# Expert tiles of a fused attention, routed-expert and gated-layer kernel: the turns of the inner rows are placed among the products

## The chip, the cores and the metric

The kernel runs on one core of one Trainium2 chip. The metric is the device time of one execution in microseconds (us); lower is better. Before the change it is 1116.9 us, the median of three runs. A time of another kernel is compared with runs of this one on the same chip.

## The reference

Three stages follow one another. Only the second is touched.

```python
state = gamma[None, :, None, None] * state + np.einsum('bhd,bhe->bhde', k[:, :, t], v[:, :, t])
y[:, :, t] = scale * np.einsum('bhd,bhde->bhe', q[:, :, t], state)
...
logits = x @ w_gate                      # x: 3072 x 512, 8 experts
e_idx = np.argmax(logits, axis=1)
for e in range(E):
    mask = e_idx == e
    h = np.maximum(x[mask] @ w1[e], 0.0) # w1[e]: 512 x 1024
    ye = h @ w2[e]                       # w2[e]: 1024 x 512
    out[mask] = gate_w[mask, None] * eom[mask, e, None] * ye
...
xn = x / rms * rms_g
g = xn @ w_gate
return (silu(g) * (xn @ w_val) @ w_out)  # inner width 1536
```

The second stage sends each of the 3072 rows through the one expert that it scores highest.

## The kernel before

Every float32 product is made of three matmuls: each operand is split into a high part in a shorter format and the low remainder, and high x high, high x low and low x high are summed in one PSUM bank. ScalarE copies out the high part (a cast), VectorE subtracts it for the low part.

The rows are sorted by expert into tiles of 128 rows. Here there are 29 real tiles, numbered 0 to 28. Tiles 0 and 1 (LEAD) are written out, since the table that steers the others is not known yet: VectorE makes it in a long chain of small operations (lines 1188 to 1291) while those two tiles run. Tiles 2 to 21 run in a hardware loop (line 695), 22 and 23 are written out, and 24 to 28 run in loops in which each pass asks whether the tile is real (lines 707 to 713). The loop on each engine has its own control instructions, and the engines meet through semaphores.

On TensorE a tile a is: `up` (line 617), 12 matmuls for inner columns 0 to 511 (g = 0) and 12 for 512 to 1023 (g = 1); `turn_hidden`, which turns the inner rows `hid` by identity matmuls, 4 for g = 0, then `turn_rows(a + 1)` (line 608), which turns the 4 blocks of the next tile's gathered rows `xg`, then 4 for g = 1 (line 632); `down_tile` (line 644), 24 matmuls, 12 for each g in the order w2h x hidh, w2l x hidh, w2h x hidl. So a tile has 48 products of 512 columns and 12 turns of 128 columns.

Around that, ScalarE makes `hid` from each half of `up` (`relu`, line 852), then `hidh` for g = 0 (line 869), `xgh` of the next tile's rows (`rows_hi`, line 859) and `hidh` for g = 1. VectorE makes `hidl` for g = 0 (line 1163), `xgl` (`rows_lo`, line 1158), `hidl` for g = 1. GpSimd gathers the rows two tiles ahead once `tile_turned` says that `xg` is free.

The weights of the next expert are split while the present one's tiles run. In the first tile of an expert ("go") ScalarE splits three pieces (line 821) between `tile_result` of the tile before and `relu(a, 0)`, and one piece at the tile's end; in the second tile ("held") the same with the four pieces of w2. VectorE makes their low parts (line 1128).

Waits of TensorE that bear on the change: `relu_done` before each `turn_hidden` half, `hTh` (hidh is there) and `hTl` (hidl is there) in `down_tile`, `rows_in` before `turn_rows`, `tileT_lo` (xgl is there) at the next tile's head.

Of the kernel before, what the change touches and what calls it, by code (L numbers as in the profile page):

```python
# [16 lines left out]
P = 128  # L17
# [14 lines left out]
SURE = TOKENS // P  # L32
# [68 lines left out]
def build(nc, q, k, v, w_gate, w_og, w1, w2, f_gate, f_val, f_out, rms_g, out):  # L101
    with ExitStack() as ctx:
# [16 lines left out]
        s = {n: ctx.enter_context(nc.semaphore(n)) for n in sem_names}  # L119
# [156 lines left out]
        def quad(b):  # L276
            return bank[b][:, :].rearrange("p (a b) -> p a b", b=P)
# [200 lines left out]
        def _(pe):  # L478
# [123 lines left out]
            def turn_rows(a):  # L602

                pe.wait_ge(s["rows_in"], 16 * (a + 1))
                if not (isinstance(a, int) and a < 1):
                    pe.wait_ge(s["tileT_lo"], a)
                for i in range(KD):
                    mm = pe.transpose(quad(XG_T)[:, i, :], xg[:, i * P:(i + 1) * P], ident)  # L608
                mm.then_inc(s["tile_turned"], 1)

            def up(a, at, g):

                if not (isinstance(a, int) and a == 0):
                    pe.wait_ge(s["relu_done"], 2 * a - 1 + g)
                terms = [(x, wt, i) for x, wt in ((xgh, w1h), (xgh, w1l), (xgl, w1h)) for i in range(KD)]
                for n, (x, wt, i) in enumerate(terms):
                    mm = pe.matmul(bank[(UP0, UP1)[g]][:, :], x[:, i, :], wt[:, ds(at + (i * FE + g * 512), 512)],  # L617
                                   start=(n == 0), stop=(n == len(terms) - 1))
                mm.then_inc(s["up_done"], 1)

            def turn_hidden(a):

                first = isinstance(a, int) and a == 0
                for g in range(2):
                    if g:
                        turn_rows(a + 1)
                    pe.wait_ge(s["relu_done"], 2 * a + g + 1)
                    if not first:
                        pe.wait_ge(s["hTl"], 2 * a - 1 + g)
                    for i in range(4):  # L630
                        f = 4 * g + i
                        mm = pe.transpose(quad((HT0, HT1)[g])[:, i, :], hid[:, f * P:(f + 1) * P], ident)  # L632
                    mm.then_inc(s["h_turned"], 1)

            def down_tile(a, at):

                if not (isinstance(a, int) and a == 0):
                    pe.wait_ge(s["tile_out"], a)
                for g in range(2):
                    for x, wt in ((hidh, w2h), (hidh, w2l), (hidl, w2h)):  # L640
                        if wt is w2h:
                            pe.wait_ge(s["hTh" if x is hidh else "hTl"], 2 * a + g + 1)
                        for f in range(4 * g, 4 * g + 4):
                            mm = pe.matmul(bank[DOWN][:, :], x[:, f, :], wt[:, ds(at + f * D, D)],  # L644
                                           start=(f == 0 and x is hidh and wt is w2h),
                                           stop=(f == KE - 1 and x is hidl))
                mm.then_inc(s["tiles_done"], 1)

            def expert_tile(a):
                at = pe.value_load(run_at[0:1, ds(a, 1)], min_val=0, max_val=HALF)  # L650
                run = pe.value_load(run_of[0:1, ds(a, 1)], min_val=0, max_val=EXPERTS - 1)
                pe.wait_ge(s["tileT_lo"], a + 1)
                pe.wait_ge(s["lo_done"], RUN * run + PER)
                for g in range(2):
                    up(a, at, g)
                turn_hidden(a)
                pe.wait_ge(s["lo_done"], RUN * run + RUN)
                down_tile(a, at)

# [8 lines left out]
            gate_logits(last)  # L668
            pe.wait_ge(s["x_out"], last)
            turn_x(last)  # L670
            up(0, 0, 1)
            ranks(last)
            turn_hidden(0)
            pe.wait_ge(s["xT_out"], UNITS)
            down_tile(0, 0)
            for a in range(1, LEAD):
                pe.wait_ge(s["tileT_lo"], a + 1)
                for g in range(2):
                    up(a, 0, g)
                turn_hidden(a)  # L680
                down_tile(a, 0)
            def turn_xn(n, halves):

# [40 lines left out]
            def weights_ready(n, m, f):  # L724

                if isinstance(n, int) and n == 0:
                    if needs_piece(m, f):
                        pe.wait_ge(s["lo_done"], RUN * runs + needs_piece(m, f))
                    else:
                        pe.wait_ge(s["early_done"], 2)  # L730

            def gate_value(n, f):
                g = NF * n + f
                if f >= 2 or not (isinstance(n, int) and n == 0):
                    pe.wait_ge(s["prod_done"], g - 1)
                for m in range(2):
                    weights_ready(n, m, f)
                    for i in range(KD):
                        if f == 0 and m == 0:
                            pe.wait_ge(s["xl_ready"], KD * n + i + 1)  # L740
                        mm = three(bank[GV[f % 2][m]][:, :], gate_parts(m, f, i),
                                   (xh[:, i, :], xl[:, i, :]), i == 0, i == KD - 1)
                mm.then_inc(s["gv_done"], 1)
# [37 lines left out]
        def _(act):  # L781
# [66 lines left out]
            def relu(a, g):  # L848
                act.wait_ge(s["up_done"], 2 * a + g + 1)
                if g == 0 and not (isinstance(a, int) and a < 1):  # L850
                    act.wait_ge(s["h_turned"], 2 * a)
                nc.scalar.activation(hid[:, g * 512:(g + 1) * 512], bank[(UP0, UP1)[g]][:, :], ACT.Relu)\  # L852
                  .then_inc(s["relu_done"], 1)

            def rows_hi(a):
                act.wait_ge(s["tile_turned"], a + 1)
                if not (isinstance(a, int) and a < 1):
                    act.wait_ge(s["up_done"], 2 * a)
                nc.scalar.activation(xgh[:], quad(XG_T), ACT.Copy).then_inc(s["tileT_hi"], 1)

            def turned_hi_parts(a):

                for g in range(2):
                    if g:
                        rows_hi(a + 1)
                    act.wait_ge(s["h_turned"], 2 * a + g + 1)
                    if g == 0 and not (isinstance(a, int) and a < 1):
                        act.wait_ge(s["tiles_done"], a + 1)
                    nc.scalar.activation(hidh[:, 4 * g:4 * g + 4, :], quad((HT0, HT1)[g]), ACT.Copy).then_inc(s["hTh"], 1)  # L869

            def tile_result(a):
                act.wait_ge(s["tiles_done"], a + 2)
# [23 lines left out]
            def expert_tile(a, numbers=None):  # L896
                is_go, is_held, turn, to = numbers or tile_numbers(a)
                tile_result(a - 1)

                with act.If(is_go):  # L900
                    split_run_hi(turn, to, range(EARLY))
                with act.If(is_held):
                    split_run_hi(turn, to, range(PER, HELD_EARLY))
                relu(a, 0)
                store_tile(a - 1)
                relu(a, 1)
                turned_hi_parts(a)
                with act.If(is_go):
                    split_run_hi(turn, to, range(EARLY, PER))
                    with act.If(act.value_load(whole[0:1, ds(a, 1)], min_val=0, max_val=1)):  # L910
                        split_run_hi(turn, to, range(PER, RUN))
                with act.If(is_held):
                    split_run_hi(turn, to, range(HELD_EARLY, RUN))
# [2 lines left out]
            evacuate_yT(UNITS - 1)  # L916
            relu(0, 0)
            evacuate_x(UNITS - 1)
            relu(0, 1)
            turned_hi_parts(0)  # L920
            for a in range(1, LEAD):
                tile_result(a - 1)
                relu(a, 0)
                relu(a, 1)
                turned_hi_parts(a)
                put_tile(a - 1, (a - 1) * P)
            exps()
# [120 lines left out]
        def _(dve):  # L1048
# [107 lines left out]
            def rows_lo(a):  # L1156
                dve.wait_ge(s["tileT_hi"], a + 1)
                v3.tensor_tensor(xgl[:], quad(XG_T), xgh[:].bitcast(F32), ALU.subtract).then_inc(s["tileT_lo"], 1)
# [5 lines left out]
                  .then_inc(s["hTl"], 1)  # L1164

            def turned_lo_parts(a):
                for g in range(2):
                    if g:
                        rows_lo(a + 1)
                    hidden_lo_part(a, g)  # L1170

            choose(UNITS - 2)
            rows_lo(0)
# [141 lines left out]
                    split_run_lo(RUN * (run + 1), to, range(HELD_EARLY, RUN))  # L1315

            for a in range(1, LEAD):
                rows_lo(a + 1)
                hidden_lo_part(a, 1)
            gates_of_rows()  # L1320
            for i in range(PRE_A, PRE):
                split_pre_lo(i)
# [312 lines left out]
```

## Time and profile before

| | |
|---|---|
| median of 3 runs | 1116.9 us (1116.73 to 1118.97) |
| time of the profiled execution | 1117.19 us |
| its span | 1115.4 us |
| TensorE busy | 1093.2 us, 98% of the span |
| VectorE, ScalarE, GpSimd busy | 441.2, 377.8, 176.9 us |
| chain that ended last | TensorE 92%, VectorE 3%, DMA 2%, issue 2% |

The profiled execution is 0.3 us above the median of the runs. Stages on the span: attention and routing to about 145 us, the expert tiles to about 514.5 us, the gated layer after that. TensorE is busy nearly throughout, so a change can give back only the short times in which it waits between its matmuls, and can lose by making it wait anew.

### The profile page before, as it was taken

The page shows a single profiled execution, that of the slowest core. Times are in us where ns is not written, and L with a number is a line of the kernel's source. Part 1 is how long each engine was busy: PE and PEld are TensorE (multiplying, and loading weights), DVE is VectorE, ACT ScalarE, POOL GpSimd, SP SyncE. Part 2 cuts the span into 40 slices and gives each one's busy share as a digit, 9 for nine tenths or more (in the row PEclk, how much of TensorE's full clock was granted, in tenths as well). Part 3 has the DMA queues.
Part 4 walks back from the last instruction along what each step waited for, and adds up shares of the span by engine and source line. Part 5 has one row for each costly group of instructions (what it writes and reads, how often), then busy time and mean ns, then how long its engine had stood idle before and what let it go on. Part 6 is the DMA issues. An engine that isn't in the chain of part 4 may idle for free.

```text
span 1115.4 us, 20314 instructions
## 1 busy us (share of the span) xinstructions
PE 1093.2 (98%) x6307; PEld 908.0 (81%) x6308; DVE 441.2 (40%) x868; ACT 377.8 (34%) x613; POOL 176.9 (16%) x245
## 2 busy tenths in 40 slices
PE   7999999999999999999999999999999999999998
PEld 6888888888888888787888888788878878887886
DVE  4777767332414425432433333423333242333222
ACT  3545435343525446432224231231133122212112
POOL 2444423322221201000000300200030011001000
PEclk9999999999999999999999999999999999999999
DMA  9999816434445533422201210111021001101001
GB/s 216 243 252 240 245 61 211 148 113 122 113 122 168 172 122 133 153 76 97 63 6 34 76 35 4 47 28 38 0 75 26 12 38 38 38 0 38 1 1 38
DMA packets 114068, 101.52 MB, mean 91 GB/s; under 512 B 81856, under 2 KB 87392, under 8 KB 114016
## 3 DMA queue, kind: packets, MB, share of 16 engines
q1 hardware_dynamic: 98752, 66.07, 22.2%
q0 software_dynamic: 8832, 26.81, 7.7%
q10 hardware_dynamic: 6432, 7.96, 2.0%
q8 instruction: 31, 0.51, 0.2%
q14 instruction: 21, 0.17, 0.1%
HBM read 76.41 MB, written 20.22 MB: 87 GB/s over the span
## 4 chain that ended last, share of the span: by engine, by line
PE 92%; DVE 3%; DMA 2%; issue 2%; ACT 1%; POOL 0%; SPq 0%; POOLq 0%; ACTq 0%; DVEq 0%
PE bank L720 14%; PE bank L722 14%; PE bank L721 14%; PE banks L644 14%; PE bank L617 14%; PE banks L720 3%; PE banks L722 3%; PE banks L721 3%; PE bank L528 2%; PE banks L514 2%; PE bank L558 1%; DMA x_rows<-x_out,slot_idx 1%; PE banks L632 1%; PE bank L608 1%; PE bank L632 1%
## 5 line engine op out<-in xcount | busy, mean ns | idle before, releaser
L1397 DVE TENSOR_TENSOR gated<-bank,sig 128x512 f32<-128x512 f32 x72 | 49.8, 692 | 344.1 <-ACT sig L1011 344.1
L1011 ACT ACTIVATE sig<-bank 128x512 f32<-128x512 f32 x72 | 43.1, 598 | 328.9 <-PE bank L722 328.9
L720 PE MATMUL bank<-xh,w1h 128*128 128x512 f32 x384 | 149.4, 389 | 0.0
L721 PE MATMUL bank<-xl,w1h 128*128 128x512 f32 x384 | 149.4, 389 | 0.0
L722 PE MATMUL bank<-xh,w1l 128*128 128x512 f32 x384 | 149.4, 389 | 0.0
L721 PEld LDWEIGHTS bank<-xl,w1h 128*128 128x128 f32 x384 | 72.1, 188 | 15.0
L722 PEld LDWEIGHTS bank<-xh,w1l 128*128 128x128 f32 x384 | 72.1, 188 | 15.0
L720 PEld LDWEIGHTS bank<-xh,w1h 128*128 128x128 f32 x384 | 72.1, 188 | 14.9
L1018 ACT ACTIVATE hh<-prod 128x512 fp32r<-128x512 f32 x72 | 45.5, 632 | 110.7 <-DVE prod L1401 110.7
L1163 DVE TENSOR_TENSOR hidl<-bank,hidh 128x512 fp32r<-128x512 f32 x29 | 20.0, 691 | 131.8 <-ACT hidh L869 131.8
L1406 DVE TENSOR_TENSOR hl<-prod,hh 128x512 fp32r<-128x512 f32 x72 | 49.9, 692 | 54.2 <-ACT hh L1018 54.2
L1598 POOL DMA_INDIRECT out_rows<-x_out,cur_idx x10 | 10.1, 1007 | 380.4 <-ACT x_out L1025 290.0
L644 PE MATMUL banks<-w2h,hidh 128*128 (+1 forms) x232 | 64.8, 401 | 0.4
L617 PE MATMUL bank<-w1h,xgh 128*128 (+1 forms) x232 | 62.7, 392 | 1.3 <-issue 1.3
L1128 DVE TENSOR_TENSOR w1l<-stage,w1h 128x1024 f32 (+1 forms) x40 | 48.1, 1232 | 39.7 <-ACT w1h L821 39.7
L644 PE MATMUL banks<-w2h,hidl 128*128 (+1 forms) x232 | 62.2, 390 | 0.0
L644 PE MATMUL banks<-w2l,hidh 128*128 (+1 forms) x232 | 62.2, 390 | 0.0
L617 PE MATMUL bank<-w1h,xgl 128*128 (+1 forms) x232 | 62.2, 390 | 0.0
L617 PE MATMUL bank<-w1l,xgh 128*128 (+1 forms) x232 | 62.0, 389 | 0.0
L852 ACT ACTIVATE hid<-bank 128x512 f32<-128x512 f32 x58 | 34.4, 594 | 79.9 <-PE bank L617 79.9
L1503 POOL DMA_INDIRECT xg<-x_rows,cur_idx x28 | 28.6, 1022 | 206.4 <-PE bank L608 204.7
L720 PE MATMUL banks<-w2h,hh 128*128 128x512 f32 x144 | 56.8, 394 | 4.4 <-DVE hl L1406 4.4
(243 smaller groups left out, 2130.6 us busy)
## 6 DMA issues: line engine op xcount, KB each, us to landing
stage<-in_moe_w SPq DMA_DIRECT2D x64, 512.0 KB, 5.6
expert_rows<-tile_o ACTq DMA_DIRECT2D x29, 256.0 KB
q_raw<-in_q SPq DMA_DIRECT2D x24, 256.0 KB, 6.0
k_raw<-in_k SPq DMA_DIRECT2D x24, 256.0 KB, 6.5
v_raw<-in_v SPq DMA_DIRECT2D x24, 256.0 KB, 4.6
stage<-stage SPq DMA_DIRECT2D x64, 64.0 KB, 2.0
stage<-in_moe_w_out SPq DMA_DIRECT2D x6, 512.0 KB, 4.1
stage<-in_moe_w_gate SPq DMA_DIRECT2D x5, 512.0 KB, 5.4
```

The source lines that it names most:

```text
L617: mm = pe.matmul(bank[(UP0, UP1)[g]][:, :], x[:, i, :], wt[:, ds(at + (i * FE + g * 512), 512)], start=(n == 0), stop=(n == len(terms) - 1))
L644: mm = pe.matmul(bank[DOWN][:, :], x[:, f, :], wt[:, ds(at + f * D, D)], start=(f == 0 and x is hidh and wt is w2h), stop=(f == KE - 1 and ...
L720: pe.matmul(out_ap, lh, rh, start=first, stop=False)
L721: pe.matmul(out_ap, lh, rl, start=False, stop=False)
L722: return pe.matmul(out_ap, ll, rh, start=False, stop=last)
L852: nc.scalar.activation(hid[:, g * 512:(g + 1) * 512], bank[(UP0, UP1)[g]][:, :], ACT.Relu)\
L1011: nc.scalar.activation(sig[:], bank[GV[f % 2][0]][:, :], ACT.Sigmoid).then_inc(s["sig_done"], 1)
L1018: nc.scalar.activation(hh[:, f % 2, :], prod[:], ACT.Copy).then_inc(s["hid_hi"], 1)
L1128: nc.vector.tensor_tensor(into[:, ds(at, PIECE)], stage[:, i % STAGE, :], hi[:, ds(at, PIECE)].bitcast(F32), ALU.subtract).then_inc(s["lo_ ...
L1397: v3.tensor_tensor(gated[:], bank[GV[f % 2][0]][:, :], sig[:], ALU.mult).then_inc(s["gated_done"], 1)
L1406: v3.tensor_tensor(hl[:, f % 2, :], prod[:], hh[:, f % 2, :].bitcast(F32), ALU.subtract)\
L1503: nc.gpsimd.indirect_dma_start(xg[:].bitcast(U32), None, x_dram, bass.IndirectOffsetOnAxis(cur_idx[:, 0:1], 0))\
```

## The change

On TensorE the 4 turns of g = 0 move from behind the `up` products into the middle of those of g = 1; the 4 turns of g = 1 move behind the first four `down` products; the turns of the next tile's rows move between the two halves of `down`. ScalarE makes `relu(a, 1)` after `hidh` of g = 0, and `rows_hi(a + 1)` last. VectorE makes `rows_lo(a + 1)` last. The bank of the turned rows is used again by the gated layer, so that layer's first use of it gets a wait. The numbers of operations are the same.

```diff
-            def up(a, at, g):
+            def up(a, at, g, between=None):
...
                 for n, (x, wt, i) in enumerate(terms):
+                    if between and n == len(terms) // 2:
+                        between()
...
             def down_tile(a, at):
 
                 if not (isinstance(a, int) and a == 0):
                     pe.wait_ge(s["tile_out"], a)
                 for g in range(2):
                     if g:
                         turn_rows(a + 1)
...
                     for x, wt in ((hidh, w2h), (hidh, w2l), (hidl, w2h)):
+                        if not g and x is hidh and wt is w2l:
+                            turn_hidden(a, 1)
...
-                for g in range(2):
-                    up(a, at, g)
-                turn_hidden(a)
+                up(a, at, 0)
+                up(a, at, 1, lambda: turn_hidden(a, 0))
                 pe.wait_ge(s["lo_done"], RUN * run + RUN)
                 down_tile(a, at)
...
+                    if isinstance(n, int) and n == 0 and GV[f % 2][m] == XG_T and f < 2:
+                        pe.wait_ge(s["tileT_lo"], extra + SURE + 1)
+                        pe.sem_inc(s["stood"], 1)
...
                 for g in range(2):
                     if g:
-                        rows_hi(a + 1)
+                        relu(a, 1)
                     act.wait_ge(s["h_turned"], 2 * a + g + 1)
...
+                rows_hi(a + 1)
...
             def turned_lo_parts(a):
-                for g in range(2):
-                    if g:
-                        rows_lo(a + 1)
-                    hidden_lo_part(a, g)
+                hidden_lo_part(a, 0)
+                hidden_lo_part(a, 1)
+                rows_lo(a + 1)
...
             for a in range(1, LEAD):
+                hidden_lo_part(a, 1)
                 rows_lo(a + 1)
-                hidden_lo_part(a, 1)
```

TensorE, tile 1, from the `up` products of g = 1 (`w1h,xgh` and so on are the three terms; `con,hid` is a turn of inner rows, `con,xg` of the next rows), before:

```order
L617 MATMUL bank<-w1h,xgh 128x512 [waits relu_done]
L617 MATMUL bank<-w1h,xgh 128x512 x3
L617 MATMUL bank<-w1l,xgh 128x512 x4
L617 MATMUL bank<-w1h,xgl 128x512 x4
L632 MATMUL bank<-con,hid 128x128 [waits hTl,relu_done]
L632 MATMUL bank<-con,hid 128x128 x3
L608 MATMUL bank<-con,xg 128x128 [waits tileT_lo,rows_in]
L608 MATMUL bank<-con,xg 128x128 x3
L632 MATMUL banks<-con,hid 128x128 [waits hTl,relu_done]
L632 MATMUL banks<-con,hid 128x128 x3
L644 MATMUL banks<-w2h,hidh 128x512 [waits hTh,tile_out]
L644 MATMUL banks<-w2h,hidh 128x512 x3
```

The same place in the changed kernel, from the fifth of those twelve products on:

```order
L619 MATMUL bank<-w1l,xgh 128x512 x2
L630 MATMUL bank<-con,hid 128x128 [waits hTl,relu_done]
L630 MATMUL bank<-con,hid 128x128 x3
L619 MATMUL bank<-w1l,xgh 128x512 x2
L619 MATMUL bank<-w1h,xgl 128x512 x4
L646 MATMUL banks<-w2h,hidh 128x512 [waits hTh,tile_out]
L646 MATMUL banks<-w2h,hidh 128x512 x3
L630 MATMUL banks<-con,hid 128x128 [waits hTl,relu_done]
L630 MATMUL banks<-con,hid 128x128 x3
L646 MATMUL banks<-w2l,hidh 128x512 x4
L646 MATMUL banks<-w2h,hidl 128x512 [waits hTl]
L646 MATMUL banks<-w2h,hidl 128x512 x3
```

Six products now stand between the first turns and the first `down` product, and the turn of the next rows (`con,xg`) follows behind the last row shown.

VectorE, end of tile 0 and the head of the chain that makes the steering table (line 1190), before:

```order
L1163 TENSOR_TENSOR hidl<-bank,hidh 128x512 [waits hTh]
L1158 TENSOR_TENSOR xgl<-bank,xgh 128x512 [waits tileT_hi]
L1163 TENSOR_TENSOR hidl<-banks,hidh 128x512 [waits hTh]
L1188 MEMSET scan_ones 128x8
L1189 MEMSET new_f 1x1
L1190 SCALAR_TENSOR_TENSOR lim_e<-bank,con 128x8
```

And in the changed kernel:

```order
L1164 TENSOR_TENSOR hidl<-bank,hidh 128x512 [waits hTh]
L1164 TENSOR_TENSOR hidl<-banks,hidh 128x512 [waits hTh]
L1159 TENSOR_TENSOR xgl<-bank,xgh 128x512 [waits tileT_hi]
L1188 MEMSET scan_ones 128x8
L1189 MEMSET new_f 1x1
L1190 SCALAR_TENSOR_TENSOR lim_e<-bank,con 128x8
```

The chain now stands behind `xgl` of tile 1's rows, which waits for their turn.

## Rows read from the trace of the kernel before

**Rows 1.** The page, busy tenths and TensorE's granted clock in 40 slices

```profile
PEclk9999999999999999999999999999999999999999
```

**Rows 2.** The chain that ended last, tile starting at 310.77: start us, us, what

```profile
310.94 5.44 PE bank L617 x24
316.38 0.44 PE bank L632 x4
...
317.25 0.47 PE banks L632 x4
...
317.74 5.69 PE banks L644 x24
```

**Rows 3.** Timeline of TensorE's weight loads, same tile: start us, us, operation

```profile
315.99 0.59 PEld L632 LDWEIGHTS bank<-con,hid 128*128 128x128 f32 x4
...
317.06 0.42 PEld L632 LDWEIGHTS banks<-con,hid 128*128 128x128 f32 x4
317.71 0.30 PEld L644 LDWEIGHTS banks<-w2h,hidh 128*128 128x128 f32 x2 [0.22 <-issue]
```

**Rows 4.** Timeline of TensorE and ScalarE, same tile: first product, relu, turns, relu

```profile
310.77 1.07 PE L617 MATMUL bank<-w1h,xgh 128*128 x4
...
313.69 0.60 ACT L852 ACTIVATE hid<-bank 128x512 f32<-128x512 f32 x1 [2.03 <-PE bank L617]
...
316.22 0.60 PE L632 MATMUL bank<-con,hid 128*128 128x128 f32 x4
316.42 0.60 ACT L852 ACTIVATE hid<-bank 128x512 f32<-128x512 f32 x1 [2.13 <-PE bank L617]
```

**Rows 5.** Timeline of TensorE and ScalarE, a held tile from its first product

```profile
298.29 1.07 PE L617 MATMUL bank<-w1h,xgh 128*128 x4
...
299.09 2.96 ACT L821 ACTIVATE w2h<-stage 128x1024 f32 x3
301.95 0.57 ACT L852 ACTIVATE hid<-bank 128x512 f32<-128x512 f32 x1
```

**Rows 6.** Line 821 in 184 to 500 us: one control operation for each piece

```profile
L821 ACTq FUSED_REGOPS  x56: 37/46/57, 186.2 to 484.1; - x56
```

**Rows 7.** Timeline of VectorE, tiles 0, 1 and 2

```profile
156.10 0.16 DVE L1190 SCALAR_TENSOR_TENSOR lim_e<-bank,con 128x8 f32<-128x8 f32 x1
...
166.75 0.69 DVE L1163 TENSOR_TENSOR hidl<-bank,hidh 128x512 fp32r<-128x512 f32 x1 [0.19 <-ACT hidh L869]
...
170.03 0.68 DVE L1163 TENSOR_TENSOR hidl<-banks,hidh 128x512 fp32r<-128x512 f32 x1
...
180.48 0.68 DVE L1163 TENSOR_TENSOR hidl<-bank,hidh 128x512 fp32r<-128x512 f32 x1
```

**Rows 8.** Timeline of TensorE, tiles 0 to 3

```profile
152.97 0.63 PE L632 MATMUL bank<-con,hid 128*128 128x128 f32 x4
...
173.00 1.19 PE L617 MATMUL bank<-w1h,xgh 128*128 x4 [0.34 <-issue]
...
185.63 1.07 PE L617 MATMUL bank<-w1h,xgh 128*128 x4
```

**Rows 9.** TensorE's own control instructions: address operations of one tile, loop's end after 28

```profile
L644 PEldq ALU_OP  x16: 32/32/32, 305.2 to 306.9; - x16
...
L713 PEldq ALU_OP  x5: 32/36/36, 510.6 to 516.2; - x5
```

**Rows 10.** The chain that ended last, tile 28 into the gated layer

```profile
514.55 2.02 issue
516.57 0.47 PE bank L720
```

**Rows 11.** Timeline of TensorE and ScalarE, tile 23 and the head of 24

```profile
436.69 1.17 PE L617 MATMUL bank<-w1h,xgh 128*128 x4
...
441.34 0.60 ACT L852 ACTIVATE hid<-bank 128x512 f32<-128x512 f32 x1
...
451.50 0.72 PE L617 MATMUL bank<-w1h,xgh 128*128 x2 [0.98 <-issue]
```

More of the change, by code:

```diff
@@ L619, in up, with turn_hidden @@
                 mm.then_inc(s["up_done"], 1)
-            def turn_hidden(a):
-                first = isinstance(a, int) and a == 0
-                for g in range(2):
-                    if g:
[L626 to L633, printed above, removed]
+            def turn_hidden(a, g):
+                pe.wait_ge(s["relu_done"], 2 * a + g + 1)
+                if not (isinstance(a, int) and a == 0):
+                    pe.wait_ge(s["hTl"], 2 * a - 1 + g)
+                for i in range(4):
+                    f = 4 * g + i
+                    mm = pe.transpose(quad((HT0, HT1)[g])[:, i, :], hid[:, f * P:(f + 1) * P], ident)
+                mm.then_inc(s["h_turned"], 1)
             def down_tile(a, at):
@@ L639, in down_tile @@
                 for g in range(2):
+                    if g:
+                        turn_rows(a + 1)
                     for x, wt in ((hidh, w2h), (hidh, w2l), (hidl, w2h)):
+                        if not g and x is hidh and wt is w2l:
+                            turn_hidden(a, 1)
                         if wt is w2h:
@@ L670, in _ @@
             turn_x(last)
-            up(0, 0, 1)
+            up(0, 0, 1, lambda: turn_hidden(0, 0))
             ranks(last)
-            turn_hidden(0)
             pe.wait_ge(s["xT_out"], UNITS)
@@ L677, in _ @@
                 pe.wait_ge(s["tileT_lo"], a + 1)
-                for g in range(2):
-                    up(a, 0, g)
-                turn_hidden(a)
+                up(a, 0, 0)
+                up(a, 0, 1, lambda: turn_hidden(a, 0))
                 down_tile(a, 0)
@@ L905, in expert_tile @@
                 store_tile(a - 1)
-                relu(a, 1)
                 turned_hi_parts(a)
@@ L918, in _ @@
             evacuate_x(UNITS - 1)
-            relu(0, 1)
             turned_hi_parts(0)
@@ L923, in _ @@
                 relu(a, 0)
-                relu(a, 1)
                 turned_hi_parts(a)
@@ L1166, in turned_lo_parts @@
             def turned_lo_parts(a):
-                for g in range(2):
-                    if g:
-                        rows_lo(a + 1)
-                    hidden_lo_part(a, g)
+                hidden_lo_part(a, 0)
+                hidden_lo_part(a, 1)
+                rows_lo(a + 1)
             choose(UNITS - 2)
```

## The prediction, made before the changed kernel was run

> **What bounds the kernel now.** I read the page first, then the chain that ended last, then the timeline of single tiles on TensorE, ScalarE and VectorE. The granted clock is full in every slice [rows 1], so no time is to be had or feared there as long as TensorE stays as dense as it is. The chain names TensorE for nearly all of the expert stage. In one tile its pieces are 5.44 us for 24 `up` products, 0.44, 0.44 and 0.47 us for three sets of 4 turns, and 5.69 us for 24 `down` products [rows 2]. So a product takes 5.44/24 = 0.2267 us and a turn 0.109 us, and a tile without any wait takes 48 x 0.2267 + 12 x 0.109 = 12.19 us. Its pieces reach from 310.94 to 317.74 + 5.69 = 323.43, 12.49 us. What can be gained is therefore 0.30 us in a tile, 29 times, 8.7 us in all. Of it 0.25 us stands at the head of `down` (5.69 against 5.44): the weight load of the first `down` product comes 0.22 us late [rows 3], because `hidh` of g = 0 is made only after the turns. Some 0.04 us stands before the turns of g = 1, whose load at 317.06 follows `relu` of g = 1, which ends at 317.02 [rows 3, 4].
>
> **The change part by part.** I count from a tile's first product. In the new order the turns of g = 0 want to start at 18 x 0.2267 = 4.08 us, `down` at 24 x 0.2267 + 0.44 = 5.88, the turns of g = 1 at 6.78, the next rows' turns at 9.03, and the tile ends at 12.19 us.
>
> *Plain tiles* (neither go nor held). `relu` of g = 0 ends at 313.69 + 0.60 - 310.77 = 3.52 us [rows 4], before 4.08. `hidh` of g = 0 ends near 5.4 us, in time for 5.88: the 0.25 us wait goes. The turns of g = 1 wait for `relu` of g = 1. That one starts 0.20 us after the last `up` product has made way (316.42, where the first turn stands at 316.22 [rows 4]), so in the new order it starts at 5.88 + 0.20 = 6.08 and ends at 6.68 us. A turn follows such an end by about 0.1 us: its load 0.04 us (317.06 after 317.02 [rows 3, 4]), and the turn after that; I take 0.11, since that set of turns took 0.03 us longer than the others for it [rows 2]. That gives 6.79 against 6.78. That is just hidden, by four products. The number of passages between products and turns rises from 2 to 6 in a tile; I put the extra four at 10 ns each, 0.04 us, from the small remainder that the pieces leave (12.49 - 12.19 - 0.25 leaves 0.05 for two passages and the load at 317.06). Gain of a plain tile: 0.30 - 0.05 = 0.25 us.
>
> *Go and held tiles.* Line 821 runs 56 times in the loop tiles [rows 6], four in a tile: 7 go and 7 held tiles. There `relu` of g = 0 stands behind three pieces: it ends at 301.95 + 0.57 - 298.29 = 4.23 us [rows 5]. With 0.11 us to the turn that is 4.34 against 4.08: a new wait of 0.26 us. Before, the other half of `up` hid it. Gain: 0.25 - 0.26, nothing.
>
> *Tiles 0 and 1, and the steering table.* This is the largest term. The chain of small VectorE operations begins at 156.10, when VectorE is free of tile 0 [rows 7]. In the new order it stands behind the low part of tile 1's rows. Their turn moves behind the first half of `down`. The turns of tile 0 began at 152.97 [rows 8]; in the new order four of them are inside `up`, so `down` begins at 153.4, and after 12 products and 4 turns (3.2 us) the rows are turned from 156.7 to 157.1; `xgh` is made by 157.9, `xgl` by 158.6 (durations 0.6 and 0.68 us as in rows 4 and 7). The chain starts at 158.6 and not at 156.1, 2.5 us later, and nothing in it gets shorter. Inside that chain stands `hidl` of tile 1, before at 166.75 to 167.44 [rows 7], now at 169.7 at its end. TensorE starts tile 1 at 159.83 and wants that `hidl` after 24 products, 4 turns, 4 products, 4 turns and 4 products, at 168.0: it waits until 169.9, 1.9 us. The second `hidl` of the tile ended at 170.71; it now comes at 172.4 (2.3 us later than before less 0.6, for `xgl` is now behind it). TensorE's loop entry followed that end by 2.3 us (173.00 against 170.71) [rows 7, 8], so tile 2 starts at 174.7, 1.7 us later than before. In tile 2 VectorE's next `hidl` was at 180.48 [rows 7], behind the rest of the table and four low parts; it is later by 2.3 us and ends at 183.5, while TensorE wants it at 174.8 + 8.16 = 182.97: 0.67 us more. Tile 3, before at 185.63 [rows 8], starts 1.7 + 0.67 - 0.25 = 2.1 us later. A loss of 2.1 us. Bounds: 0 if the chain were not gated, 2.5 + 0.7 if nothing absorbed it.
>
> *Tiles 3 to 22*: 9 plain x 0.25 = 2.2 us gained; 11 go or held: 0.
>
> *Tile 23* is held and ScalarE makes two more operations first: its `relu` ends at 441.34 + 0.60 - 436.69 = 5.25 us [rows 11], so the turns wait 1.3 us. Most of that was slack, since the head of tile 24 waits for TensorE's own control instructions (0.98 us "issue" [rows 11]). These run later by what follows. Loss 0.4 us.
>
> *TensorE's control instructions.* In one tile 16 address operations run from 305.2 to 306.9 [rows 9], 0.113 us apart, the last 8.6 us after the tile's first product at 298.29 [rows 5], and the loop's end follows. In the new order the last eight follow `hidh` of g = 1, which is there at about 8.1 us, so the last comes at 8.9 us, 0.3 us later. In the hardware loop this is covered. Where the control instructions are what TensorE waits for, it costs 0.3 us and the tile's own gain is lost. Such places are the head of tile 27 and the gated layer's head, where five passes over tiles that may not be real run from 510.6 to 516.2 and TensorE stands idle for 2.02 us [rows 9, 10]. Tile 26 is held: +0.5. Tile 28: +0.3. Tiles 24, 25, 27: -0.45. Together a loss of 0.4 us. The gated layer's new wait is for something made 5 us before: nothing.
>
> **Sum**: +2.1 - 2.2 + 0 + 0.4 + 0.4 = +0.7 us. The profiled execution would be 1117.9; on the median of the runs, 1117.6 us.
>
> The step on control instructions rests on what the rows show: they do not run freely ahead, for TensorE stands 2.02 us for them [rows 10]. The Trainium skill, Perfetto Trace Analysis, in its part on the instruction lifecycle, says that an engine's instruction that waits for a semaphore is pushed into a wait queue and that the sequencer is then ready to fetch the next. That speaks against my step; rival B is the case in which it holds here, with its time from the rows.
>
> **The rivals.**
> *A: the gain arrives nearly whole.* The table's delay is absorbed and the 15 tiles that are neither go nor held gain 0.25 us each, 3.8 us: 1113.1; with the late `relu` absorbed too, 29 x 0.25 = 7.3 us: 1109.6. Against it stands the plain arithmetic of rows 5 and 7. Chance 0.08.
> *B: waits of matmuls do not hold up the control instructions behind them.* Then the later `hidh` delays no loop end: the losses of tiles 23, 26 and 28 (0.4 + 0.5 + 0.3 us) are gone and tile 28 keeps its 0.25: 0.7 - 1.45 = -0.8, 1116.1. For it: nothing in the rows shows the hold directly; against it: the 2.02 us. Chance 0.12.
> *C: the turns of g = 1 are late in every tile, slower.* Their cover is 4 products, 0.907 us, and by my count they are 0.01 us late. If their weight load must come as early as the one at 315.99, 0.23 us before its turn at 316.22 [rows 3, 4], they start at 6.68 + 0.04 + 0.23 = 6.95 and each of 29 tiles waits 0.17 us, 0.16 more than I take: +4.6 us, 1122.2. It decides (beyond 0.2%) from 1.5/29 = 0.05 us in a tile. For it: these turns now follow products, as the load at 315.99 does; against it: there the load was simply free to go early. Chance 0.16.
> *D: my forecast,* between 1115.8 and 1119.4, for errors of 0.06 us in each of 29 tiles. Chance 0.64.
>
> **How the numbers follow.** A measurement of this kernel can tell a change from none at about 0.2%, 2.2 us. The forecast and B lie within it. Faster by more: A, 0.08, and a little of B, together 0.10. Slower by more: C 0.16 and the upper end of D, together 0.20. Same: 0.70. The range leaves out A and the upper half of C: 1115.0 to 1121.0.
>
> **What the profile would show.** Right: `down` pieces of 5.4 us without an issue wait; in held tiles a wait of about 0.25 us before line 630's first turns and none in plain ones; tile starts 12.2 to 12.3 us apart in plain, 12.5 in go and held tiles; a wait on `hidl` of near 2 us in tile 1 and 0.7 in tile 2; tile 3 at 187.7; the issue wait before the gated layer 2.6 and not 2.02 us. Wrong: tiles all 12.2 us apart (A), turns of g = 1 waiting on `relu` everywhere (C), tile 3 before 186.

## The result, and the profile of the changed kernel

The changed kernel took 1133.6 us in the median of four runs (1131.05 to 1135.48), the kernel before 1116.8 us beside it: a ratio of 1.0143, 95% interval 1.0121 to 1.0164. It is slower by 1.4%. The forecast was 1117.6 us, which is no change that can be told, and its range went from 1115.0 to 1121.0. The profiled execution took 1131.05 us against 1117.19, 13.9 us more. It ran at the full granted clock; the other three had 0.997 or 0.998 as their mean, which is most of what they took longer.

First the chain that ended last, in a plain tile, against [rows 2] (start us, us, what):

```profile
408.30 4.08 PE bank L619 x18
412.38 0.44 PE bank L630 x4
412.82 1.38 PE bank L619 x6
414.20 0.91 PE banks L646 x4
415.11 0.44 PE banks L630 x4
415.55 1.84 PE banks L646 x8
417.38 0.44 PE bank L608 x4
417.82 2.74 PE banks L646 x12
420.56 0.45 PE bank L619 x2
```

The pieces follow each other without a gap: 12.26 us from tile to tile, where the forecast had 12.24 (12.49 less 0.25). Neither the wait at the head of `down` nor one before the turns of g = 1 is there. So rival C, the turns of g = 1 late in every tile, is out. The loss is elsewhere. TensorE's waits, summed (engine and line, what it waited for: us, times, longest):

```profile
PE bank L630 <- ACT hid L854: 15.3, 13, 2.1
PE bank L487 <- POOL k_s L1445: 7.5, 1, 7.5
PE banks L719 <- DVE hl L1406: 4.4, 5, 0.9
PE bank L719 <- issue: 2.5, 1, 2.5
PE banks L646 <- DVE hidl L1164: 1.8, 2, 1.5
PE bank L619 <- issue: 1.5, 2, 0.9
```

The first and the fifth row are new: in the same list of the kernel before, no turn of inner rows and no `down` product waits for ScalarE or VectorE. The fifth, the wait for `hidl`, is the one that was forecast for tiles 1 and 2. The first was forecast as 0.26 us in a go or held tile and is far more. Line 630's first turns, those of g = 0 inside `up`, wait 13 times for `hid`, the `relu` of g = 0. Taken from the starts of the matmuls (the distance to the turn, less the 0.227 us of a product), all 29 waits are 17.6 us (the list counts from the modelled end of the product before, and so shows less): 0.73 us in the usual go tile (1.03, 0.10 and 1.30 in three others), 1.70 to 1.74 in the held tiles of the loop, 1.29 in tile 23, 2.30 in tile 26. The forecast had 0.26 in each but tile 23. Why the `relu` is so late stands in ScalarE's timeline from the end of a go tile into a held one, whose first product stands at 251.30:

```profile
246.45 0.60 ACT L871 ACTIVATE hidh<-banks 128x512 fp32r<-128x512 f32 x1 [0.77 <-PE banks L630]
248.82 0.60 ACT L861 ACTIVATE xgh<-bank 128x512 fp32r<-128x512 f32 x1 [1.78 <-PE bank L608]
249.32 1.05 ACT L823 ACTIVATE w1h<-stage 128x1024 f32 x1
253.10 0.60 ACT L879 ACTIVATE tile_o<-banks 128x512 f32<-128x512 f32 x1 [2.73 <-issue]
253.61 2.01 ACT L823 ACTIVATE w2h<-stage 128x1024 f32 x2
255.52 1.04 ACT L823 ACTIVATE w2h<-stage 128x1024 f32 x1
256.47 0.58 ACT L854 ACTIVATE hid<-bank 128x512 f32<-128x512 f32 x1
```

`tile_o`, the copy of the last tile's sums, could start when these are complete. In the kernel before it starts 0.29 us into a tile, which here would be 251.6. It starts at 253.10, after 2.73 us in which ScalarE waits for no other engine ("issue"), and everything behind it is late with it. The chain that ended last tells what fills that time:

```profile
248.82 0.05 ACT xgh L861
...
249.26 0.27 ACTq L913
...
250.50 0.05 ACTq L968
250.58 0.29 ACTq L894
250.91 0.16 ACTq L894
251.20 0.28 ACTq L895
251.51 0.15 ACTq L895
251.80 0.28 ACTq L896
252.11 0.15 ACTq L896
252.39 0.29 ACTq L897
252.71 0.15 ACTq L897
...
253.10 0.06 ACT tile_o L879
```

These are ScalarE's own control instructions (ACTq): the test of `whole` (L913), the loop's branch (L968), and the four numbers of the next tile, `go`, `held`, `run_of` and `next_at` (L894 to L897), 0.6 us each. They begin only when `xgh` (L861), the copy of the next rows, has started at 248.82, and from there to `tile_o` it is 4.28 us. (At the end of a plain tile, which has neither the piece nor the test of `whole`, it is 3.28 us, from 235.74 to 239.02.) The change made this copy ScalarE's last operation of a tile, and it waits for a turn that the change put into the middle of `down`. So `tile_o` is 1.5 us late in this held tile and 0.5 us late in the go tile before it (239.02, where the tile started at 238.20). With the forecast's own 0.26 us that makes waits of 1.76 and 0.78 us, for the measured 1.71 and 0.72.

Where the 13.9 us went, by the first product of a tile in the two traces (for the forecast's parts):

| part | before | after | difference | forecast |
|---|---|---|---|---|
| tiles 0 to 2 | 39.65 | 41.80 | +2.2 | +2.1 |
| tiles 3 to 22 | 251.06 | 259.70 | +8.6 | -2.2 |
| tile 23 | 14.81 | 15.74 | +0.9 | +0.4 |
| tiles 24 to 28 and the stand behind them | 65.07 | 68.94 | +3.9 | +0.4 |

The sum is 15.6 us. Tile 0 began 1.5 us earlier in the trace of after (144.44 against 145.98), and the gated layer lasts the same within 0.2 us. Where tile 0 begins differs from trace to trace without any edit ahead of it: experiments 6 and 12, below, have 144.56 and 145.27 for the order of the kernel before.

### The profile page after: what moved, and what is told of

Its sections match the earlier page's. It is cut to its first block, busy times and chain, and to the rows that moved or that the text cites. A ratio compares the mean times of both kernels' runs of the same rounds, so it can differ in the third digit from the quotient of the medians.

```text
span 1129.3 us, 20316 instructions
## 1 busy us (share of the span) xinstructions
PE 1090.0 (97%) x6307; PEld 901.1 (80%) x6308; DVE 446.0 (39%) x868; ACT 387.5 (34%) x613; POOL 181.6 (16%) x245
## 4 chain that ended last, share of the span: by engine, by line
PE 82%; DVE 4%; ACTq 4%; issue 4%; ACT 3%; DMA 1%; DVEq 0%; POOL 0%; SPq 0%; POOLq 0%
PE bank L719 14%; PE bank L720 14%; PE bank L721 14%; PE banks L646 10%; PE bank L619 8%; PE banks L719 3%; PE banks L721 3%; PE banks L720 3%; PE bank L528 2%; PE banks L514 2%; PE bank L558 2%; PE bank L630 1%; PE bank L608 1%; PE banks L507 1%; PE bank L566 1%
## 5 line engine op out<-in xcount | busy, mean ns | idle before, releaser
L619 PE MATMUL bank<-w1l,xgh 128*128 (+1 forms) x232 | 69.4, 401 | 0.0
L646 PE MATMUL banks<-w2l,hidh 128*128 (+1 forms) x232 | 65.2, 402 | 0.0
L1129 DVE TENSOR_TENSOR w2l<-stage,w2h 128x1024 f32 (+1 forms) x40 | 47.5, 1223 | 27.1 <-ACT w2h L823 27.1
L721 PE MATMUL banks<-w2h,hl 128*128 128x512 f32 x144 | 56.1, 390 | 0.0
```

The source lines that it names most:

```text
L721: return pe.matmul(out_ap, ll, rh, start=False, stop=last)
L1129: nc.vector.tensor_tensor(into[:, ds(at, PIECE)], stage[:, i % STAGE, :], hi[:, ds(at, PIECE)].bitcast(F32), ALU.subtract).then_inc(s["lo_ ...
```

## The experiments

Two theories. **T1**: TensorE's stands in go and held tiles come from ScalarE's control instructions, which wait behind the late copy of the next rows. **T2**: they come from the new place of the first turns together with the three pieces of weights ahead of `relu`, whatever stands last on ScalarE. T3, in experiments 5 and 9, is T1 without the control instructions: the late copies alone would pass their lateness on. Times of tiles are distances of first products in the profiled execution.

**1. rows_ahead: the rows' turn back ahead of `down`.** The other two moves stay.

```diff
-                    if g:
+                    if not g:
                         turn_rows(a + 1)
...
                     if g:
                         relu(a, 1)
+                        rows_hi(a + 1)
...
-                rows_hi(a + 1)
```

(VectorE likewise: `rows_lo` between its two hidden parts.)

> The changed kernel with the next rows' turn put back ahead of the down products (up with the turns of g=0 inside, rows' turn, 4 down products, turns of g=1, the rest); ScalarE and VectorE make the rows before the second half of the turned hidden part. Theory T1 (the stands of TensorE in go and held tiles come from ScalarE: its control instructions wait behind the copy of the next rows, which the change made its last and late operation of a tile): that copy starts near +6.7 us of a tile instead of +9.7 and the last operation ends near +8.3 instead of +10.2, so the control instructions are ready before the tile ends, tile_o starts at once, and the waits before the first turns fall from 0.73 (go) and 1.72 us (held) to about 0.26: 17.6 - 14 x 0.26 = 13.9 us less; the steering table starts early again, 2.1 us less: 1131.05 - 16.0 = 1115.0 in the profiled execution, plain tiles 12.25 us apart. Rival T2 (the stands come from the place of the first turns and the three pieces alone, whatever is behind them on ScalarE): waits stay 0.7 and 1.7 us, and only the table's share comes back: 1129.

Measured: 1119.4 us, ratio to before 1.0013 (1.0004 to 1.0022). The waits fell to 0.18 to 0.21 us in the go and held tiles of the loop (all 29 together 3.3 us, of which 1.10 in tile 23). Tiles of the loop: plain 12.27 to 12.29 us, go and held 12.51 to 12.55. This is as T1 has it; T2 is out. A held tile's head in this trace:

```profile
298.53 0.60 ACT L878 ACTIVATE tile_o<-banks 128x512 f32<-128x512 f32 x1 [3.12 <-PE banks L646]
299.03 2.96 ACT L823 ACTIVATE w2h<-stage 128x1024 f32 x3
301.90 0.58 ACT L854 ACTIVATE hid<-bank 128x512 f32<-128x512 f32 x1
```

`tile_o` now waits for the products and no longer for "issue": it starts 0.30 us after the tile's start at 298.23, as in the kernel before. Tiles 0 to 2 took 39.93 us, 0.3 more than before: 1.9 of the 2.2 us came back. The expected 1115.0 was missed, by 6.6 us in the profiled execution (1121.56 us, the slowest of the eleven), mostly behind tile 23: tiles 24 to 28 and the stand behind them took 67.4 us, 2.3 more than before, and then the clock fell:

```profile
515.40:518.40 3.00, 0.01 (x1) 0.04 (x1) 0.00 (x0) 0.60 (x1) 0.00 (x0) 0.83 0.05 18
518.40:523.40 5.00, 5.00 (x12) 3.94 (x13) 0.00 (x0) 1.28 (x1) 0.00 (x0) 0.50 0.12 43
523.40:530.00 6.60, 6.60 (x29) 5.41 (x28) 1.79 (x3) 1.67 (x3) 0.00 (x0) 0.94 0.01 2
```

(stretch, its length, busy us and count of PE, PEld, DVE, ACT and POOL, granted clock, share and GB/s of the transfers.) TensorE stood still for 2.99 us, and the next 5 us ran at 0.50, the 1.2 GHz level: 12 matmuls where full speed has some 22.

**2 and 3. The dose: the rows' turn after 8 or 16 `down` products instead of 12.**

```diff
                     for x, wt in ((hidh, w2h), (hidh, w2l), (hidl, w2h)):
+                        if not g and x is hidl:
+                            turn_rows(a + 1)
```

(for 16: `if g and x is hidh and wt is w2l`; the call at `if g` goes.)

> The changed kernel with the next rows' turn 4 products (0.91 us) earlier, after 8 down products instead of 12; the order on ScalarE and VectorE is unchanged. T1: the copy of the rows and all that stands behind it on ScalarE come 0.91 us earlier; held tiles wait 1.72 - 0.91 = 0.81 us, go tiles 0.26 (the floor that the three pieces set), 7 x 0.91 + 7 x 0.46 = 9.6 us less: 1121.4. T2: no change in the stands, 1131 less some 0.9 us for the table: 1130.

> The changed kernel with the next rows' turn 4 products (0.91 us) later, after 16 down products instead of 12. T1: every go and held tile waits 0.91 us more, 1.63 and 2.63 us, 14 x 0.91 = 12.7 us, and the table comes 0.9 us later: 1144.5. Plain tiles stay near 12.25 us, since xgl would end at +11.9 us against 12.25. T2: no change in the stands of go and held tiles, at most 1 us for the table: 1132.

Measured: at 8, 1122.9 us (ratio 1.0050, 1.0035 to 1.0066) and 1121.43 in the profiled execution, with waits of 0.18 (go) and 0.79 to 0.84 us (held) in the loop, where T1 had 0.26 and 0.81. All 29 waits are 9.6 us less, as T1 had it. At 16, 1154.0 us (1.0320, 1.0304 to 1.0336), with waits of 1.41 and 2.41 us. These are less than T1's 1.63 and 2.63, yet the time rose more, by 20 to 26 us and not 13. Some 10 us is in the waits. The granted clock had a mean of 0.993 over the profiled 1155.7 us, which alone is 8 us. The expectation also missed two things: plain tiles lasted 12.42 to 12.56 us and not 12.25, for the next tile now starts just behind its rows' low part (`xgl` ends 12.14 us into tile 14, the next starts at 12.49), and tiles 0 to 2 took 3.3 us more than in the changed kernel, where T1 had 0.9. The later the turn, the longer the stand: T1's mechanism, with a further price behind long stands.

**4. two_pieces: one piece less ahead of the first `relu`** (`EARLY = 2`, `HELD_EARLY = PER + 2`).

> The changed kernel with two instead of three pieces of weights ahead of the first relu in go and held tiles, on ScalarE and VectorE; the third goes to the pieces at the tile's end. T1: relu of g=0 comes one piece (about 0.95 us) earlier, so go tiles wait nothing, 7 x 0.73 = 5.1 us less; but the piece now stands with the late ones, behind the rows' copy and ahead of the control instructions of the next tile, so in held tiles tile_o starts 0.95 us later and the wait stays near 1.7 us: 1126. T2 (only the count of pieces ahead of relu matters): go tiles wait nothing and held tiles 0.77 us, 5.1 + 6.7 = 11.8 us less: 1119.3.

Measured: 1122.8 us (1.0042, 1.0026 to 1.0057), between the two expectations. Go tiles wait 0.01, held ones of the loop mostly 0.95 to 0.98. So T1's second half was wrong, that the piece would come back whole in front of the next `tile_o`. From the start of `xgh` to that of `tile_o` it is 4.46 us here (247.85 to 252.31) and 4.28 in the changed kernel (248.82 to 253.10): a piece more at the tile's end costs the control instructions 0.18 us and not its 0.95. So corrected, T1 gives held tiles 1.72 - 0.95 + 0.18 = 0.95 us, as measured. They run beside a copy that is under way; what holds them is a copy that *waits*.

**5 and 6. The same control instructions where there is slack and where there is none.**

```diff
                 to = act.value_load(next_at[0:1, ds(a, 1)], min_val=0, max_val=HALF)
+                act.value_load(real[0:1, ds(a, 1)], min_val=0, max_val=1)
```

(one such line in the changed kernel, three in the kernel before.)

> The changed kernel with one more number read on ScalarE in each expert tile (a fifth value load beside go, held, run_of and next_at; its value isn't used). One such load takes about 0.6 us of ScalarE's control instructions. T1 (control instructions behind the late copy of the rows make tile_o late): tile_o starts 0.6 us later in every tile; in the 14 go and held tiles this goes straight into the wait before the first turns (1.3 and 2.3 us), 14 x 0.6 = 8.4 us more, 1139.5 in the profiled execution; plain tiles stay 12.26 us. T3 (the copy of the rows and the pieces are late for themselves, their lateness passed on by the copies on ScalarE, and control instructions run beside it): no change, 1131.

> The kernel before with three more numbers read on ScalarE in each expert tile, 1.8 us of control instructions. T1: there the last wait of a tile on ScalarE ends at +7.1 us, the control instructions had 1.57 us of slack, and relu of g=0 ends at 4.23 us where the turns want it at 5.44: tile_o comes 0.2 to 0.3 us later and all is hidden, within 1 us of the kernel before, 1117 to 1118. If control instructions cost ScalarE's time wherever they stand, as T1 without its slack would have it: 22 x 1.8 = 40 us at most, 14 x 0.6 = 8 us at least.

Measured: three loads more in the kernel before, 1117.5 us, ratio 1.0003 (0.9994 to 1.0012): nothing. They took 1.6 us, about the slack: behind a go tile `tile_o` starts 0.41 us into the tile (247.24, the tile from 246.83) and not 0.29. One load more in the changed kernel: 1145.9 us, ratio 1.0255 (1.0239 to 1.0270), 12.3 us more in the medians and so more than either expectation. The waits rose by 0.59 us in go and held tiles (1.32 and 2.27 to 2.36), 8.0 us over all 29: near T1's 8.4, and T3's none is out. The rest is mostly the clock, with a mean of 0.994. Some held tiles with their 2.3 us stand lasted 14.6 us, others 16.3:

```profile
253.68:261.20 7.52, 5.36 (x26) 4.23 (x25) 3.84 (x4) 4.37 (x6) 2.46 (x3) 1.00 0.43 136
261.20:264.80 3.60, 3.60 (x12) 2.77 (x12) 0.80 (x2) 0.77 (x2) 0.00 (x0) 0.53 0.00 0
264.80:269.94 5.14, 5.14 (x28) 4.25 (x27) 2.06 (x3) 2.26 (x3) 1.50 (x2) 1.00 0.32 108
```

In the 3.6 us of the middle row TensorE had the 1.2 GHz level and made 12 matmuls.

**7. rows_alone: the kernel before with the rows' turn moved, nothing else** (on TensorE, ScalarE and VectorE as in the change; both sets of hidden turns ahead of `down`).

> The kernel before with one part of the change alone: the next rows' turn, and its parts on ScalarE and VectorE, behind the first half of the down products; the turns of the hidden rows stay together ahead of down. By the order: without the rows' turn between them, the turns of g=1 find relu of g=1 ending at 5.65 + 0.60 = 6.25 us of the tile, 0.48 us after they want to start (5.88), and hidh of g=0, behind that relu, is ready at 6.85, so down starts near 7.15; a plain tile lasts 13.0 instead of 12.49 us, 29 x 0.54 = 15.7 us. The table's delay adds 2 us: 1135. The late relu of g=0 in go and held tiles (5.0 and 5.7 us) hides in that wait. If the parts of the change add up one by one instead, this part has the whole stand of go and held tiles and leaves plain tiles at 12.49: 1117.2 + 13.6 + 2 = 1133, told apart by the distance of plain tiles.

Measured: 1136.0 us (1.0166, 1.0151 to 1.0182), plain tiles 12.94 to 13.01 us, as worked out. This part alone costs as much as the whole change (1.0143, 1.0121 to 1.0164): in the kernel before, the rows' turn also covered the `relu` of g = 1. Now the turns of g = 1 wait for it 22 times, 5.5 us by the profile's list, where they never waited before. Held tiles of the loop lasted 13.33 to 13.37 us, with waits of 0.37 us, so their late `relu` did not hide wholly.

**8. rows_ahead_two: experiments 1 and 4 together.**

> rows_ahead and two_pieces together: the turns of g=0 among the up products, the rows' turn ahead of down, the turns of g=1 after four down products, and two pieces ahead of the first relu. In rows_ahead go and held tiles last 12.52 and plain ones 12.28 us. T1: relu of g=0 comes a piece (0.95 us) earlier, at 3.5 us, before the turns want it: go and held tiles 12.28 too, 14 x 0.24 = 3.4 us less than rows_ahead's 1118.4 to 1119.4: 1115 to 1116, 0.2% under the kernel before. Rival: the third piece, now at the tile's end, delays what follows it on ScalarE or VectorE (tile 23 and the tiles behind the loop), and nothing is gained: 1119.

Measured: 1115.95 us (0.9988, 0.9979 to 0.9997). Tiles 3 to 21 all last 12.27 to 12.29 us, and the 29 waits sum to 0.3 us. The time is 0.1% under the kernel before and no more, since tiles 24 to 28 and the stand behind them still take 67.4 us for 65.1.

**9. result_first: `tile_o` ahead of the numbers,** in the changed kernel.

```diff
+                if not numbers:
+                    tile_result(a - 1)
                 is_go, is_held, turn, to = numbers or tile_numbers(a)
-                tile_result(a - 1)
+                if numbers:
+                    tile_result(a - 1)
```

> The changed kernel with tile_result(a - 1), the copy that frees the sums' bank, issued on ScalarE ahead of the four numbers of tile a instead of behind them (tiles 3 to 22 and those behind 23). The numbers are then read while tile_o is being copied. T1: in held tiles the pieces start where tile_o started before, 0.51 us earlier, and the wait falls from 1.72 to 1.2 us; in go tiles tile_o starts with the end of the last tile's products and the wait falls from 0.73 to the floor of 0.26: 7 x 0.51 + 7 x 0.46 = 6.8 us less, 1124.3 in the profiled execution. If the control instructions didn't count (T3): no change, 1131.

Measured: 1161.8 us (1.0410, 1.0394 to 1.0426), far on the other side. I had thought that the numbers would be read while `tile_o` waits. Instead (chain that ended last, around the start of a held tile at 258.79):

```profile
256.21 2.75 PE banks L646 x12
258.99 0.04 ACTq L878
259.03 0.05 issue
259.08 0.06 ACT tile_o L879
259.14 0.03 issue
259.17 0.29 ACTq L894
```

The wait for the sums stands on a control instruction (ACTq L878), which runs at 258.99, when the products are done; the first number (L894) is read at 259.17, behind `tile_o` at 259.08. ScalarE takes its control instructions in order and none passes the one that waits. The waits are now 2.4 to 2.7 us in the loop's go and held tiles, 33.7 us over all, and the mean granted clock 0.987. The pieces begin at 262.01, 3.22 us into the tile and not 0.80 as in the kernel before [rows 5]; with the 0.26 us that makes 2.68 us, for the measured 2.62. So my expectation, which applied T1 to `xgh` and forgot it for `tile_o`, was wrong by 37.5 us, part of them the clock's. T1's rule taken to `tile_o` gives the waits, and T3 is out once more.

**10. no_g1_move: rows_ahead with the turns of g = 1 ahead of `down` too.**

> rows_ahead with the turns of g=1 put back ahead of down: up with the turns of g=0 inside, then the rows' turn, the turns of g=1 and the 24 down products. It measures what covers relu of g=1. That relu ends 0.80 us after the last up product's end and a turn follows it by 0.11 us; the rows' turn covers 0.44 us of the 0.91, so TensorE waits 0.47 us in each tile: 12.28 + 0.45 = 12.7 us in plain tiles, 29 x 0.45 = 13 us more than rows_ahead's 1119.4: 1132. Rival: relu of g=1 is covered by its own early start and nothing is lost: 1119.

Measured: 1129.4 us (1.0113, 1.0098 to 1.0129). Plain tiles 12.74 us, 0.46 more than rows_ahead, with the turns of g = 1 waiting for `hid`: the rival is out. The total rose by 10 us and not 13, for tiles 24 to 27 lasted as long as in rows_ahead (51.8 us); something else sets their length.

**11. old_order_behind: rows_ahead_two with the old order in tiles 24 to 28.**

```diff
                 with pe.If(pe.value_load(real[0:1, ds(a, 1)], min_val=0, max_val=1)):
-                    expert_tile(a)
+                    expert_tile(a, True)
```

(`True`: turns of g = 0, rows, turns of g = 1, then 24 products; on ScalarE `relu` of g = 1 ahead of `hidh`.)

> rows_ahead_two, with the order of the kernel before (both sets of turned hidden rows and the next rows together ahead of down) in tiles 24 to 28 alone. In rows_ahead_two these tiles last 12.77, 12.74, 13.56 and 12.80 us and the gated layer's first product waits 2.99 us, against 12.61, 12.55, 12.56, 12.68 and 2.02 before. Theory T4 (behind the last wait of a tile, for hidl of g=1, TensorE still needs 3.4 us for its control instructions; that hidl ends at 9.35 us in the new order and at 8.66 in the old, and 9.35 + 3.39 = 12.74): tiles of 12.5 to 12.6 us again and 2.0 us before the gated layer, 1.5 + 1.0 = 2.5 us less: 1113.5 in the median, 0.3% under the kernel before. Rival (these tiles are longer because two pieces or the later copies on ScalarE hold them): nothing is gained, 1116.

Measured: 1111.7 us, ratio 0.9952 (0.9938 to 0.9966), granted clock 1.0 in all five runs: 0.5% faster than the kernel before, and faster than the changed one. Tiles 24 to 27 are back at 12.50 to 12.63 us, and the stand behind tile 28 at 1.95:

```profile
504.95 4.76 PE banks L646 x21
509.71 1.95 issue
511.66 0.47 PE bank L723
```

That is T4, and the tiles from 24 on with the stand gained the expected 2.5 us (67.4 to 64.9 us). T4 also fits the other traces. From the end of the second `hidl` to the next tile's first product it is 3.37 to 3.49 us in tiles 24, 25 and 27 of rows_ahead, rows_ahead_two and the changed kernel, and from that of tile 28 to the gated layer's first product 5.97 to 6.20 us in these, the kernel before and this run, while that `hidl` of tile 28 ends anywhere from 8.65 to 9.39 us into the tile. Tile 26 lasts some 0.8 us longer than this in rows_ahead and rows_ahead_two, which T4 doesn't explain. The median gained 4.3 us and not 2.5; the runs of rows_ahead_two had mean clocks of 0.997 and 0.998, and 0.002 to 0.003 of 1116 us is 2 to 3 us, enough for the rest. In tiles 3 to 22 the gain of the moved turns is whole: 246.4 us for 251.1 in the kernel before.

**12. before_two_pieces: a control,** the two pieces in the kernel before.

> The kernel before with two instead of three pieces ahead of the first relu, nothing else: a control for old_order_behind, which was 0.5% faster than the kernel before. In the kernel before relu of g=0 ends at 4.23 us in go and held tiles and the turns want it at 5.44, so an earlier relu is worth nothing: loop tiles stay 12.49 to 12.55 us apart and the time stays at 1117. Rival (the gain comes from the two pieces alone, for example in tile 23, where the pieces are late by more): up to 14 x 0.25 = 3.5 us less, 1113.5.

Measured: 1116.5 us, 0.9995 (0.9986 to 1.0004): the pieces alone do nothing. The 0.5% needs the moved turns.

## Why the prediction was wrong

**The step that failed** is *Go and held tiles*: "There `relu` of g = 0 stands behind three pieces: it ends at [...] 4.23 us". That time was read from the kernel before, with the head of the tile taken as unchanged. But `tile_o`, the pieces and `relu` stand behind ScalarE's control instructions, which stand behind its last waiting copy. The prediction put that at nothing without saying so. In the kernel before, the last such copy started at +7.1 us of a tile, and the control instructions had some 1.5 us of slack: at the end of a go tile they were done at 246.9, and `tile_o` started at 248.50, with the products. Experiment 6 used it up with no loss. The change made `xgh`, at +9.8 us, the last, and used up the slack. The waits were 0.73 and 1.72 us, not 0.26. With the rows' turn put back ahead of `down` the same arithmetic holds: 12.51 to 12.55 us in experiment 1 for the forecast's 12.5. I had used this very rule for TensorE and not asked it of ScalarE.

- *Plain tiles*: right, 12.26 for 12.24 us; the turns of g = 1 hidden.
- *Tiles 0 and 1, steering table*: right, in mechanism and size. The table's chain began 12.65 us behind tile 0's first product for 10.12 before, 2.5 us later as forecast. TensorE waited for `hidl` 1.7 us in tile 1 and 0.55 in tile 2 (the first `w2h x hidl` product stands at 9.91 and 8.72 us of the tile, in a plain one at 8.17), forecast 1.9 and 0.67; +2.2 us for +2.1. Experiment 1 took 1.9 of it away.
- *Tiles 3 to 22*: +8.6 us for -2.2, the failed step: the waits there sum to 12.6 us, where 11 of 0.26 were forecast.
- *Tile 23*: the wait was 1.29 us for 1.3, and in part by luck: in experiment 1, where the failed step is out of the way, it was 1.10. The tile with the stand behind it lost 0.9 us for 0.4, so less of the wait was slack than the forecast took.
- *TensorE's control instructions*: the stand before the gated layer was 2.53 us for 2.6. The +3.9 us of the last part are mostly the waits of tiles 25 and 26, 1.30 and 2.30 us, the failed step again. Behind tile 26 TensorE waited 0.5 us more, for `w2l`, VectorE's low part of the last piece: it follows ScalarE's, and that the late `xgh`. The forecast had no such term.
- *Rival B* is refuted as worded by experiment 9 for ScalarE, and for TensorE by experiment 11: the later `hidl` did lengthen the stand, 2.99 us in rows_ahead_two and 1.95 with the old order. The sentence from the Trainium skill (Perfetto Trace Analysis, instruction lifecycle) on the sequencer being ready for the next instruction does not describe what the control instructions do here. In experiment 9 the wait stood on a control instruction, which the sentence does not speak of; but where it stands on the copy itself nothing passes either: in a plain tile of the changed kernel `relu` of g = 0 waits for `up`, with ScalarE idle before it for 1.49 us, and starts at 228.857 us, and the first control instruction behind it, of the load of `row_at` (L886), starts at 228.863.

What stays open: when the clock falls, for stands of 2.3 us went both with and without a fall; and the longer tile 26 of experiments 1 and 8.

## What to carry to other kernels

Before an operation is moved later on an engine, ask what follows it there up to the next thing that another engine wants, and count the value loads and branches among it: they are not on the engine's busy time but they start only when the last waiting operation has started. The move costs nothing while that chain has slack (here 1.5 us) and the whole excess beyond. And a short independent piece of work, such as the rows' turn, may be the cover of two waits: see which before it goes.

## What the runs showed of the hardware

- A number read into a register on ScalarE took 0.28 us for the load and 0.15 for the operation behind it, with the rest some 0.6 us. Four of them and the loop's branch took 2.8 us in the changed kernel (250.15 to 252.93), nearly a quarter of a tile.
- Control instructions ran beside a copy under way (L886 at 254.30 in the changed kernel, under the pieces of 253.61) but not past one that waited (L886 at 228.863, behind the `relu` of 228.857).
- Behind stands of 2 to 3 us TensorE's granted clock fell to the 1.2 GHz level for several microseconds in some cases (products 0.427 us apart for 0.227) and not in others. The kernel before, with its 2.02 us stand, shows means of 1.0 and of 0.998 in different runs of one program (beside experiments 6 and 12), 1 to 2 us apart, and in the profiled execution of experiment 6 the gated layer's first 4 us, behind the stand, ran at 0.57.
